# Four scatters behind the last score-value products, and the first expert's direct products ahead of its loaded rows

## The reference

```python
# attention: B, H, S, D = 2, 8, 768, 48
for t in range(S):
    cur = np.einsum('bhd,bhe->bhde', u[None] * kt, vt)
    y[:, :, t] = np.einsum('bhd,bhde->bhe', rt, state + cur)
    state = w[None, :, :, None] * state + np.einsum('bhd,bhe->bhde', kt, vt)
x = y.transpose(0, 2, 1, 3).reshape(1536, 384)
# experts: E = 8, F = 1024, capacity 384
logits = x @ w_gate
expert_idx = np.argmax(logits, axis=1)
gate_w = softmax(logits)[expert_idx]
# disp[e, pos] = x[i] for the first 384 tokens i of expert e, in order
h = np.maximum(disp @ w1[e], 0); y = h @ w2[e]
out[i] = gate_w[i] * y[expert_idx[i], pos[i]]
# dense: 384 -> 2048 -> 384
h = x @ w_in;  g = h - np.tanh(h);  return g @ w_out
```

## Time and profile before

| | us |
|---|---|
| median of 3 runs | 408.28 |
| lowest, highest | 408.23, 409.46 |
| the profiled execution, in all | 410.51 |
| its span, first to last instruction | 408.8 |
| its mean granted clock | 0.98 |
| PE busy | 384.9 (94%) |
| DVE, ACT, POOL busy | 214.2, 180.9, 155.7 |

### The profile page before, as it was taken

One profiled execution on the slowest core, in us unless ns is written; L12 is line 12 of the kernel. 1 busy time (PEld: TensorE's weight loads), 2 busy tenths in 40 slices (PEclk: granted clock), 3 DMA queues, 4 the chain that ended last, 5 costly groups with the idle time before them and its releaser, 6 DMA issues.

```text
span 408.8 us, 10468 instructions
## 1 busy us (share of the span) xinstructions
PE 384.9 (94%) x3738; PEld 373.1 (91%) x3739; DVE 214.2 (52%) x453; ACT 180.9 (44%) x486; POOL 155.7 (38%) x132
## 2 busy tenths in 40 slices
PE   7999898698999999999999899999999999999991
PEld 7777687598999999999999899999999999999991
DVE  7667978574555655555465356615252434343340
ACT  5553456434564665756656454533022313231220
POOL 3966665435877742715517051541002000110002
PEclk9999999689999999999999999999999999999997
DMA  7989986444849478576684527000000000010001
GB/s 246 271 251 269 249 211 220 141 149 154 264 162 285 150 249 261 189 253 192 224 284 158 182 79 226 6 21 38 0 0 19 38 0 0 0 58 0 0 0 65
DMA packets 41541, 56.85 MB, mean 139 GB/s; under 512 B 3584, under 2 KB 39104, under 8 KB 41504
## 3 DMA queue, kind: packets, MB, share of 16 engines
q1 hardware_dynamic: 35936, 46.23, 36.9%
q10 hardware_dynamic: 3600, 5.31, 4.1%
q0 software_dynamic: 1968, 4.83, 3.1%
HBM read 46.23 MB, written 10.13 MB: 138 GB/s over the span
## 4 chain that ended last, share of the span: by engine, by line
PE 58%; issue 18%; POOL 13%; DVE 4%; DMA 2%; ACT 2%; another core or an unknown queue 1%; POOLq 0%; DVEq 0%; SPq 0%; ACTq 0%
POOL w_lo L460 11%; PE ring L1065 9%; PE ring L1067 9%; PE ring L1066 9%; PE pO L1317 8%; PE pO L1316 8%; PE pY L1189 2%; POOL token_of_rank L521 2%; PE ring L1205 2%; PE pA L1140 2%; PE pD L1094 1%; DVE At L880 1%; PE pY L1174 1%; PE pX L1084 1%
## 5 line engine op out<-in xcount | busy, mean ns | idle before, releaser
L460 POOL TENSOR_TENSOR w_lo<-raw_weights,w_hi 128x768 fp32r<-128x768 f32 x40 | 73.5, 1846 | 84.6 <-ACT w_hi L580 84.3
L1007 DVE SCALAR_TENSOR_TENSOR minus_tanh<-square,ring 128x384 f32<-128x384 f32 x64 | 35.5, 554 | 93.5 <-ACT square L730 79.1
L580 ACT ACTIVATE w_hi<-raw_weights 128x768 fp32r<-128x768 f32 x80 | 67.1, 848 | 28.5 <-DMA raw_weights<-w 28.4
L730 ACT ACTIVATE square<-ring 128x384 f32<-128x384 f32 x64 | 31.4, 491 | 94.7 <-DVE h_hi L1017 53.8
L1065 PE MATMUL ring<-yT_hi,w_hi 128*128 x192 | 65.0, 339 | 1.7 <-DVEq L1002 1.7
L1316 PE MATMUL pO<-w_hi,h_hi 128*128 128x384 f32 x192 | 64.9, 338 | 0.0
L1317 PE MATMUL pO<-w_lo,h_hi 128*128 128x384 f32 x192 | 64.8, 338 | 0.0
L1066 PE MATMUL ring<-yT_lo,w_hi 128*128 x192 | 64.8, 338 | 0.0
L1067 PE MATMUL ring<-yT_hi,w_lo 128*128 x192 | 64.8, 338 | 0.0
L1065 PE MATMUL ring<-xT_hi,w_hi 128*128 128x224 f32 x192 | 52.9, 275 | 1.6 <-issue 1.1
L849 DVE TENSOR_TENSOR w_lo<-raw_weights,w_hi 128x768 fp32r<-128x768 f32 x40 | 42.4, 1073 | 22.3 <-ACT w_hi L580 18.7
(11 more groups left out here) (158 smaller groups left out, 744.1 us busy)
## 6 DMA issues: line engine op xcount, KB each, us to landing
raw_weights<-w SPq DMA_DIRECT2D x80, 384.0 KB
x_by_slot<-x ACTq DMA_DIRECT2D x9, 576.0 KB, 4.4
x_expert<-x_by_slot SPq DMA_DIRECT2D x8, 576.0 KB
kv<-kv_by_token SPq DMA_DIRECT2D x22, 192.0 KB, 4.2
rkT<-rk_by_feature SPq DMA_DIRECT2D x18, 192.0 KB, 5.1
rkT<-rk_by_feature SPq DMA_DIRECT2D x3, 512.0 KB, 4.5
x_expert<-x_by_slot SPq DMA_DIRECT2D x1, 384.0 KB
x_by_slot<-x,sloti POOLq DMA_INDIRECT x12, 4.1
```

The costliest lines, as they stand in the source:

```text
L460: pool.tensor_tensor(lo, unit_raw(2, k), hi.bitcast(F32), ALU.subtract).then_inc(w2_ready, 1)
L580: act.activation(hi, unit_raw(what, k), ACT.Copy).then_inc(w1_hi if what == 1 else w2_hi, 1)
L730: act.activation(sq[:, i % 2, :], ring[i % 4][:, 0:CAP], ACT.Square, scale=THIRD ** 0.5, accum_out=sqsum[:, bass.ds(t * (2 * FC) + i, 1)]) ...
L1007: dve.scalar_tensor_tensor(out=nt[:, i % 2, :], in0=sq[:, i % 2, :], scalar=1.0, in1=ring[i % 4][:, 0:CAP], op0=ALU.subtract, op1=ALU.mult ...
```

## The change

In GpSimd's program, step 11 gets one more wait: for `y_full` of step 11, the signal of the last score-value products, behind the iota and ahead of the scatters of tiles 4 to 7. In PE's program three unused products are put between the last transposes and the last logits; the unused products behind the position products of tiles 10 and 11 go from two to five; and the direct products of tiles 10 and 11 are put ahead of the wait for the loaded rows, so that the loaded rows' products come last and give `ring_full`.

```diff
@@ GpSimd
                     pool.iota(slots[:, :], [[1, CAP]], base=0, channel_multiplier=0,
                               allow_small_or_imprecise_dtypes=True).then_inc(slots_ready, 1)
+                    pool.wait_ge(y_full, STEPS)
                 for i in SENT.get(n, []):
                     scatter(i)
@@ PE
             def loaded(c, k, cols):
                 at = slice(k * P + cols.start, k * P + cols.stop)
-                pe.matmul(ring[c][:, at], xe[:, k, c * P:(c + 1) * P], ident[:, cols], start=False, stop=False,
-                          skip_group_check=True)
+                return pe.matmul(ring[c][:, at], xe[:, k, c * P:(c + 1) * P], ident[:, cols], start=False, stop=True,
+                                 skip_group_check=True)
             near, far = slice(0, NARROW), slice(NARROW, CAP)
+            keep_warm(3, ones[:, :], pA[:, 0, 0, :])
             logits(STEPS - 1)
...
             direct(9, 2, near, False, False)
-            keep_warm(2, ones[:, :], pX[:, 0:P])
+            keep_warm(5, ones[:, :], pX[:, 0:P])
+            for c in range(KD):
+                direct(10, c, near, False, False)
+                direct(11, c, near, False, False)
             pe.wait_ge(xe_in, 16)
             for c in range(KD):
                 loaded(c, 0, slice(0, P))
-                loaded(c, 1, slice(0, NARROW - P))
-            for c in range(KD):
-                direct(10, c, near, False, False)
-                direct(11, c, near, False, True).then_inc(ring_full, 1)
+                loaded(c, 1, slice(0, NARROW - P)).then_inc(ring_full, 1)
```

## The result

The changed kernel took 414.89 us, the median of 4 runs (413.15 to 417.67), against 408.25 for the kernel before (4 runs, 405.47 to 409.46): ratio 1.018, 95% interval 1.010 to 1.026. Slower, where 407.3 was forecast. A ratio is taken over the executions within 1.5% of the fastest of their kernel, which can leave out more of one kernel than of the other, while a median takes all of them, so both are given.

The account below looks back on a forecast made before the run. TensorE (PE), busy 94% of the span, was taken as the bound, so time won before the first expert product counts at the end. -2.03 + 0.42 + 0.66 = -0.95 off the 408.28 median gave 407.3 us, range 406.2 to 409.7.

Parts of the forecast that it names:

- The sum: Total ahead of the first expert product: -2.03 + 0.42 + 0.66 = -0.95 us, giving 407.3 us.
- The unused products: Six added on PE: three before tile 11's logits cost 0.42 us, three ahead of the direct products 0.66.
- a 0.50 at 87: Sign in the profile's clock row, half clock at 87 us, under which the forecast would be wrong by most.
- its rival: Clock stays at half until the loaded rows: adds 3.6 us, 410.9; chance 0.05 together with late rows.
- The gain of 2.03: Idle time ahead of step 11's last attention tile goes, starting PE's chain 2.03 us earlier.
- with y_full at 74.06 the attention tile starts when the weight piece ends: Last attention tile on VectorE starts at 75.45, not 77.48, once scatters 4 to 7 move: 2.03 us.
- The first rival: Late signals before the last attention tile come from recording, so only the products' cost remains: 409.3 us, chance 0.28.
- The later scatters cost nothing: Scatter 4 starts 1.73 us later, yet expert 0's loaded rows still land with 2.3 us of cover left.
- in the old order of products PE would have wanted the rows at 85.7 and had none: With loaded products before direct ones, no cover would remain for rows landing at 85.1 to 85.9 us.
- no new wait for the loaded rows: Sign ahead of the first expert product: PE wants the rows at 88.2 us, after they land, and doesn't wait.
- the order of the products: Direct products of tiles 10 and 11 before loaded ones: same twenty-four passes, no added wait, priced zero.
- The rival of an early clock: Full clock from the first direct product on, gain bounded to about 1.6 us: 405.7 us, chance 0.13.

Follow-up runs that it names:

- x2: Kernel before plus six unused products in a branch expert 0 does not enter, so only code behind it shifts; chip A, ratio 1.017.
- x4: Kernel before plus the six executed unused products alone, without the new wait or new order; chip A, ratio 1.021.
- y2: The changed kernel itself, measured again beside the kernel before; chip B, ratio 1.010.
- v1: The changed kernel itself, measured again beside the kernel before; chip D, ratio 0.998.
- v4: Same kernel as x2, the kernel before with code shifted by six never-executed products; chip D, ratio 1.007.
- x1: Changed kernel with six products cut from a branch expert 0 does not enter, putting later code back in place; chip A, ratio 1.015.
- x3: Kernel before plus the one GpSimd wait for y_full ahead of scatter 4; chip A, ratio 1.013.
- y1: The kernel before, unchanged, timed against itself; chip B, ratio 1.001.
- z1: Same kernel as x1, the changed kernel with code back in place; chip C, ratio 0.997.
- z2: Changed kernel without its six unused products, keeping the GpSimd wait and new order, code in place; chip C, ratio 0.996.
- z4: Kernel before plus the six executed unused products, with six products cut from the branch not entered to keep code in place; chip C, ratio 1.007.
- v2: Same kernel as x1, the changed kernel with code back in place; chip D, ratio 0.987.
- v3: Same kernel as z2, the changed kernel without its six unused products; chip D, ratio 0.993.
- u1: Same kernel as z2, the changed kernel without its six unused products; chip A, ratio 1.003.
- u2: Same kernel as x1, the changed kernel with code back in place, measured again; chip A, ratio 1.010.
- y4: Changed kernel plus 58 unused products (232 instructions) in the branch expert 0 does not enter; chip B, ratio 1.006.
- z3: Changed kernel with twelve products cut from the branch expert 0 does not enter, making its code shorter; chip C, ratio 0.998.

## Why the prediction was wrong, step by step

**The sum lacked a term: where the added code puts the code behind it.** "The unused products" were priced by their passes, 0.42 and 0.66, and nothing else. They also moved expert 0's products by 24 instructions against the pieces in which PE's program arrives. All six traces with that shift (after, x2, x4, y2, v1, v4) have 1.34 to 1.92 us of idle time behind product 2 and the clock at 0.50 within 2 us of its end. All eleven with the code where it was (before, x1, x3, y1, z1, z2, z4, v2, v3, u1, u2) have 0.62 or less behind product 14, and none a fall of the clock there. By time the shift alone cost 0.7% (v4) and 1.7% (x2), 3 to 7 us, or 2.8 and 3.8 us by the medians. This is shown: x2 and v4 execute what the kernel before executes. What I can't show is that the idle time, and not something with it, lets the clock fall; y4, u2, z3 and x3 have falls behind waits of 4.08, 3.07, 2.51 and 1.93 at other places, which speaks for it. The closing sentence that the forecast would be wrong by most with "a 0.50 at 87" had some of the size (its rival adds 3.6 us) and no mechanism: the fall came at 92, behind another wait.

**The gain of 2.03 was that of one kind of chip.** The step "with y_full at 74.06 the attention tile starts when the weight piece ends" was right wherever the signal was late: without the wait the tile stood behind 2.03, 1.67 and 2.14 us of "remote" (before, z4, v4), with it behind none (z1, z2, z3, v1, v2, v3). On chips A and B no trace of any kernel has a "remote", with the wait or without, and nor has the result's profile of the kernel after, which therefore says nothing of this term. There the term is zero, and the first expert product of the unchanged kernel (90.43 in y1) was as early as the changed one's. I took my baseline from one trace and laid it beside a median of other executions. The profile of the kernel after agrees with the forecast down to the first expert product by luck: it has no late signals of its own, and is laid beside a trace that has them.

**The first rival had the gain right where no signal is late, and the wrong reason.** "The late signals are not in the timed runs" gave 409.3, no gain from the hole and the products' cost; it lacked the term of the code's place as the forecast did. Its ground was that recording makes the hole. Every profile is recorded alike, and the hole comes in the first trace of the kernel before and on chips C and D, not on A and B, so recording alone doesn't make it; the times go with this (v3 0.993, z2 0.996, u1 1.003). The rule of the Trainium skill that I put behind it ("NOTIFIC — the notification-queue block", section 7.1) isn't borne out as the cause here. Nor does the other one ("SBUF — State Buffer", "SBUF: two separate sides") tell what moving the scatters does: on chip D z2's edit (v3), which is the wait and the order together, gained 0.7%.

**"The later scatters cost nothing" followed the chain one link too short, and took the wait from one trace.** It put scatter 4 off by 1.73 us; in the six traces with a slow stretch ahead, GpSimd stood 4.27 to 5.19 us. It priced the rows of expert 0, and these were never waited for by more than 0.3 us in a trace with the wait and the new order. It named scatters 8 to 11 as queued behind, and left out that expert 1's rows wait for them. That cost 0.32 to 3.07 us in three traces of the twelve with the wait and the new order, and nothing in the others. x3, which has the wait and the old order, waited 1.93 us for expert 0's rows, as the sentence that "in the old order of products PE would have wanted the rows at 85.7 and had none" has it; x4, old order and no wait, waited 0.53.

**What held.** Scatter 4 at 73.77 (forecast 74.22), no "remote" at the tile on the chips with late signals, no new wait for the loaded rows, the order of the products at no cost that shows. The products' passes, 1.1 us or 0.3%: z1 over z2 0.1%, u2 over u1 0.7%, v2 over v3 -0.6%: 0.1% on the average, which can't be told from the term or from nothing. The rival of an early clock appears in u2 and z3 (ten passes in 2.14 us), and its gain went into the wait for expert 1's rows.

**What stays open.** On chip A, x1 (1.015), u2 (1.010) and x3 (1.013) are slower than their terms allow with the code in place. By the medians they are 1.008, 1.001 and 1.009, so how much there is to explain in x1 and u2 is itself not settled. The wait for expert 1's rows in u2, and for expert 0's in x3, is a cause for part of it; x1's one trace has neither, and how often they come in the timed executions isn't known. x3 ran at a mean clock of 0.941 to 0.968 in its seven executions, where the kernel before on that chip ranged from 0.956 to 0.989, and no run tells why. Why signals are late on some chips wasn't tried, and no run holds the idle time for code while the clock stays up, so the two costs of the shift can't be told apart by time.

The changed kernel less its six unused products (z2, v3, u1) is the best version of it here: 0.996, 0.993 and 1.003, by the medians 0.994, 0.992 and 0.998.

## What to carry to other kernels

An instruction added to an engine's program moves all the code behind it against the pieces in which it is fetched; where a branch lands shortly before the end of a piece, the fetch isn't covered. Look for idle time put down to "issue" at the same count of instructions behind a branch, and test with code that is never executed. Count on a gain of a microsecond or two only where the wait stands in the traces of more than one chip, and price a new wait also in a trace where the stage ahead ran slow. And follow a delayed transfer to its second consumer, not only to its first.

## What the runs showed of the hardware

PE's idle time for code ended 1.8 to 2.4 us after the first expert product started, whether two products or fourteen stood between (v4: 93.23 and 95.05; v2: 89.56 and 92.00); the piece fetched is 0.02 MB. With 232 more instructions in the branch not entered, 4.08 us of idle time stood ahead of the first product behind it (y4). Late signals go with the chip: x2 and v4 are one kernel, and VectorE's last attention tile stood behind no "remote" on chip A (x2) and behind 2.14 us on chip D (v4); y1 on B had none either and the same kernel's first trace 2.03. ScalarE stood 2.98 to 3.09 us for tile 8's transposes in all eight traces of C and D, beside a string of indirect DMA issues on GpSimd.
